# Attention feeding a gated mixer and a channel block: the scores of the second head get PSUM banks of their own

## The reference

```python
    scores = scale * np.matmul(q, k.transpose(0, 1, 3, 2))      # q, k: (4, 8, 576, 64)
    mask = pos[:, None] // 64 >= pos[None, :] // 64
    scores = np.where(mask, scores, -1000000000.0)
    scores = scores - np.max(scores, axis=-1, keepdims=True)
    attn = np.exp(scores)
    attn = attn / (np.sum(attn, axis=-1, keepdims=True) + 1e-09)
    return np.matmul(attn, v)
```

## Time and profile before

| | us |
|---|---|
| median of 3 runs | 778.47 |
| lowest and highest run | 778.45, 778.65 |
| the profiled execution | 780.42 |
| its span, first to last instruction | 778.6 |
| TensorE busy in it | 768.2 |
| mean granted clock of TensorE, share of 2.4 GHz | 0.997 |

### The profile page before, as it was taken

One profiled execution on the slowest core, in us unless ns is written; L12 is line 12 of the kernel. 1 busy time (PEld: TensorE's weight loads), 2 busy tenths in 40 slices (PEclk: granted clock), 3 DMA queues, 4 the chain that ended last, 5 costly groups with the idle time before them and its releaser, 6 DMA issues.

```text
span 778.6 us, 14021 instructions
## 1 busy us (share of the span) xinstructions
PE 768.2 (99%) x5024; PEld 674.3 (87%) x5024; DVE 475.2 (61%) x963; ACT 364.9 (47%) x970; POOL 388.7 (50%) x508
## 2 busy tenths in 40 slices
PE   7999999999999999999999999999999999999998
PEld 6877899779987799879988998888998898889986
DVE  4776745465553755448867676788556687444435
ACT  4886765546554555433543333453423345333431
POOL 3787665234352344313555456465555457454641
PEclk9999999999999999999999999999999999999999
DMA  7344331312214120040362311003100001300002
GB/s 237 135 168 150 106 116 48 102 61 78 77 48 136 41 75 18 21 155 14 122 190 89 114 55 55 28 0 122 55 28 2 1 0 41 122 1 1 0 1 82
DMA packets 38148, 56.38 MB, mean 72 GB/s; under 512 B 3136, under 2 KB 20544, under 8 KB 38080
## 3 DMA queue, kind: packets, MB, share of 16 engines
q1 hardware_dynamic: 38080, 55.49, 22.0%
HBM read 46.04 MB, written 9.44 MB: 71 GB/s over the span
## 4 chain that ended last, share of the span: by engine, by line
PE 97%; DVE 1%; ACT 1%; issue 1%; POOL 0%; POOLq 0%; ACTq 0%; DVEq 0%
PE psum L1393 25%; PE psum L1394 25%; PE psum L1395 25%; PE psum L1306 7%; PE psum L1355 5%; PE psum L1374 3%; PE psum L1379 3%; PE psum L1359 2%; PE psum L1472 1%; ACT probs L808 1%; PE psum L1445 1%; PE psum L1428 1%; DVE neg_max L1035 1%; PE psum L1426 0%; DVE mix_buf L1097 0%
## 5 line engine op out<-in xcount | busy, mean ns | idle before, releaser
L762 POOL TENSOR_TENSOR wp_r<-block,wp_r 128x256 fp32r<-128x256 f32 x168 | 133.8, 804 | 168.3 <-ACT wp_r L939 166.0
L1210 DVE TENSOR_TENSOR sums<-psum,sums 128x384 f32<-128x384 f32 x216 | 113.6, 553 | 105.9 <-PE psum L1395 105.2
L967 ACT ACTIVATE h_r<-sums 128x384 fp32r<-128x384 f32 x96 | 50.4, 525 | 228.9 <-PE psum L1395 119.1
L694 POOL TENSOR_SCALAR probs<-probs,row_inv 128x64 f32<-128x64 f32 (+4 forms) x160 | 87.4, 566 | 111.6 <-DVE row_inv L1046 111.6
L1395 PE MATMUL psum<-w_r,h_r 128*128 128x512 f32 x288 | 114.2, 397 | 0.0
L1394 PE MATMUL psum<-w_r,h_r 128*128 128x512 f32 x288 | 113.7, 395 | 0.0
L1393 PE MATMUL psum<-operand,wp_r 128*128 128x384 f32 x336 | 113.2, 337 | 0.2 <-DVE sums L1210 0.2
L1394 PE MATMUL psum<-operand,wp_r 128*128 128x384 f32 x336 | 113.1, 336 | 0.0
L1395 PE MATMUL psum<-operand,wp_r 128*128 128x384 f32 x336 | 112.4, 334 | 0.0
L1393 PE MATMUL psum<-w_r,h_r 128*128 128x512 f32 x288 | 111.9, 389 | 0.0
L808 ACT ACTIVATE probs<-psum,neg_max 64x64 f32<-64x64 f32 (+4 forms) x160 | 83.0, 527 | 53.7 <-DVE neg_max L1035 52.6
(11 more groups left out here) (121 smaller groups left out, 1592.1 us busy)
## 6 DMA issues: line engine op xcount, KB each, us to landing
qk_raw<-qk SPq DMA_DIRECT2D x32, 576.0 KB, 4.4
block<-w_ch SPq DMA_DIRECT2D x32, 256.0 KB, 4.0
y_res<-y_scratch SPq DMA_DIRECT2D x18, 256.0 KB, 4.1
out<-y_res SPq DMA_DIRECT2D x18, 256.0 KB, 2.1
v_raw<-vN SPq DMA_DIRECT2D x16, 256.0 KB, 2.8
y_scratch<-mix_buf SPq DMA_DIRECT2D x16, 256.0 KB, 2.1
y_ring<-y_scratch SPq DMA_DIRECT2D x16, 256.0 KB, 2.7
w_raw<-w_in SPq DMA_DIRECT2D x8, 256.0 KB, 4.5
```

The source lines that it names most:

```text
L694: pool.tensor_scalar(probs[:, n % 2, c], probs[:, n % 2, c], row_inv[:, n % 2, AT[t]:AT[t] + 1], 1.0, ALU.mult, ALU.mult).then_inc(normed, 1)
L762: pool.tensor_tensor(wp_lo[:, n % WP], w1[i % BLOCKS][:, WEIGHT[j]], wp_hi[:, n % WP].bitcast(F32), ALU.subtract).then_inc(wp_lo_done, 1)
L1210: dve.tensor_tensor(dst, product_bank(i, j), other, ALU.add).then_inc(c_summed, 1)
```

## The change

The scores of head 1 get banks 3 to 5 in place of 0 to 2 (`start += 3 * 512`), and the corner of head 0's own tile moves to bank 6, of head 1's to bank 7. `score_head(1)` is issued right behind `score_head(0)`, and no longer waits for the exponentials of head 0. VectorE sets eight corners in place of four. Behind the two sets of scores come eight identity matmuls with 64 output rows in place of six with 128. The loop issues no scores in head 0's turn.

Two waits are new in the turn of head 0. The transposes of tile 3 go to bank 7, where head 1's own scores lie now, and wait for their exponential. The transposes of tile 2 go to bank 3, and wait for all ten exponentials of heads 0 and 1 (`exped` at 10). Nothing changes from head 2 on, but for the place of the own tile in heads 0 and 1.

```diff
--- before.py
+++ after.py
@@ -344,7 +344,9 @@
 
         def transposed_free(pe, n, t):
 
-            if t == 3 and H < n + 1 < HEADS:
+            if t == 2 and n == 0:
+                pe.wait_ge(exped, 2 * NT)
+            if t == 3 and (n == 0 or H < n + 1 < HEADS):
                 pe.wait_ge(exped, NT * (n + 1) + 1)
             elif t == 2 and n >= H:
                 pe.wait_ge(t_copied_dve, len(DVE_TILES) * n + 1)
@@ -367,13 +369,15 @@
         def score_of(n, t):
             flat = psum.rearrange("p a n -> p (a n)")
             if t == 0:
-                return (m_bank if n <= H else t_bank)[BLOCK:P, 1, 7 * BLOCK:8 * BLOCK]
+                bank = t_bank[:, 0, :] if n == 0 else m_bank[:, 1, :] if 1 < n <= H else t_bank[:, 1, :]
+                return bank[BLOCK:P, 7 * BLOCK:8 * BLOCK]
             start = {4: 0, 3: KEYS[4], 2: KEYS[4] + KEYS[3], 1: KEYS[4] + KEYS[3] + KEYS[2]}[t]
+            start += 3 * 512 if n == 1 else 0
             return flat[:, start:start + KEYS[t]]
 
         def unseen():
 
-            return [score_of(0, t)[0:BLOCK, KEYS[t] - BLOCK:KEYS[t]] for t in TILES[1:]]
+            return [score_of(n, t)[0:BLOCK, KEYS[t] - BLOCK:KEYS[t]] for n in range(2) for t in TILES[1:]]
 
         def parts(t):
             return slice(BLOCK, P) if t == 0 else slice(0, P)
@@ -1315,7 +1319,7 @@
             def score_head(n):
 
                 pe.wait_ge(q_scaled, n + 1)
-                if n >= 1:
+                if n >= 2:
                     pe.wait_ge(exped, NT * n)
                 if n > H:
                     pe.wait_ge(t_copied_act, len(ACT_TILES) * (n - 2) + 2)
@@ -1445,14 +1449,16 @@
                     pe.matmul(t_bank[:, 0, 0:P], ident[:, :], ident[:, :], start=True, stop=True)
 
             keep_warm(10)
-            pe.wait_ge(masks_set, 4)
+            pe.wait_ge(masks_set, 8)
             pe.wait_ge(consts_set, 5)
             score_head(0)
-            keep_warm(6)
+            score_head(1)
+            for _ in range(8):
+                pe.matmul(t_bank[0:BLOCK, 0, 0:P], ident[:, 0:BLOCK], ident[:, :], start=True, stop=True)
             for n in range(HEADS):
                 for step in range(STEPS):
                     if step == 0:
-                        if n + 1 < HEADS:
+                        if 1 <= n < HEADS - 1:
                             score_head(n + 1)
                         if n >= 1:
                             attend(n - 1)
```

## The result

The changed kernel is slower. The median of its 13 runs is 780.55 us (779.65 to 781.63), that of 13 runs of the kernel before beside them 778.65 us (778.35 to 782.17), and the ratio is 1.0019 with a 95% interval of 1.0012 to 1.0027. That is 1.9 us, and outside the range of the prediction (776.5 to 779.9). The runs of before aren't all alike: nine took 778.35 to 779.02 us, and four 780.46 to 782.17, about as long as the runs after the change.

The account below looks back on a forecast made before the run. TensorE, busy 99% of the span, was taken as the bound, with idle stretches and its clock as levers. A chain gain of 0.84 less 0.65 given back left 0.19 us, so 778.47 became 778.3 us; range 776.5 to 779.9.

Parts of the forecast that it names:

- What bounds the kernel, and where the change acts: Whole span: TensorE busy 99%, so only its few idle stretches, two near the start, and its clock can move the time.
- Part 1, the chain: Head 1's scores move up, its wide maximum follows at 12.06, not 12.90; TensorE's release comes 0.84 us earlier.
- Parts 2 and 3, what is given back: Head 0's transposes start at 13.0; seven now stand between the release and head 2's scores, giving back 0.65 us.
- Part 4, filler and masks: Eight identity matmuls behind the first two heads' scores and four more memsets fall in idle time and cost nothing.
- Cost nothing; the cover ends there: Filler ahead of head 0's transposes: even at the slow price it would end at 13.9, transposes at 15.2, before 15.89.
- equal clock: Head 2's scores: the clock falls at about the same place as before, leaving 0.19 us gained, 778.3 us; chance 0.58.
- rival B: Head 2's scores: the change puts there a fall that unprofiled runs of before lack; 1.47 us slower, 779.9 us; chance 0.15.
- Rival A: Head 2's scores: the clock no longer falls and they take 2.03 us; gain 1.85 us, 776.6 us; chance 0.18.

Follow-up runs that it names:

- experiment 4: Kernel before with only the wait for all ten exponentials added ahead of head 0's tile 2 transposes; median 779.35 us, ratio 1.0014.
- experiment 6: Changed kernel plus five identity matmuls in bank 0 between the first three tiles' transposes and the wait for all exponentials; median 778.96 us, ratio 0.9995.
- Experiment 5: Changed kernel with twelve in place of eight identity matmuls behind the scores of heads 0 and 1; median 780.18 us, ratio 1.0010.
- 1: Kernel before with twelve for six identity matmuls behind head 0's scores and four behind head 0's transposes; median 778.84 us, ratio 0.9997.
- 2: Changed kernel with twelve for eight identity matmuls ahead of head 0's transposes and five in bank 0 before the wait; median 778.29 us, ratio 0.9993.
- 7: Changed kernel with both idle stretches filled and eight in place of ten identity matmuls at the start; median 778.22 us, ratio 0.9989.
- 9: Kernel before with both idle stretches filled and eight in place of ten identity matmuls at the start; median 778.52 us, ratio 0.9999.
- 11: Changed kernel, idle stretches filled, eight matmuls at the start, weight loads queued behind head 5's and 6's q and k loads; median 778.07 us, ratio 0.9985.
- the tenth kernel: Kernel before without the six identity matmuls behind head 0's scores; median 778.82 us, ratio 1.0006.

## Why the prediction was wrong, point by point

**What bounds the kernel, and where the change acts.** Right. All of it lies ahead of head 3's scores: the rest takes 755.1 us before and after.

**Part 1, the chain.** Right in mechanism and size. VectorE's program order kept the own maximum of head 1 at 4.15 us behind the wide maxima of head 0 (12.19 less 8.04), before 4.16 (11.83 less 7.67). The release came 9.06 - 8.23 = 0.83 us earlier, forecast 0.84.

**Parts 2 and 3, what is given back.** Right in mechanism, the size a little small. The first transposes wait for the normalised tile until 13.43, 13.06 without the shift of 0.37, forecast 13.0. The seven transposes cost 17.01 - 16.27 = 0.74 us, forecast 0.65, and 0.73 to 0.76 in experiment 4. The prediction took 0.12 us for each of the two wide ones out of a pipelined row of ten; behind a wait the two take 0.34 until the next group can start. The net gain is 0.83 - 0.74 = 0.09 us, forecast 0.19.

**Part 4, filler and masks.** The filler took 1.96 us in idle time, as worked out, and the eight memsets 0.63, forecast 0.66:

```profile
0.80 0.63 DVE L1018 MEMSET psum<- 64x64 f32 x8 [0.80 <-PEq L1550]
```

But the step "Cost nothing; the cover ends there" priced filler by TensorE's time alone. The gap that it leaves open costs more: with five more matmuls there (experiment 6) the median is 778.96 us against 780.55, on another chip, and no fall is left.

**The step that failed: the clock.** The prediction saw that the stretch from 12.2 to 16.54 was thinner than before, and forecast a fall over the scores of head 2. It came, in 13 of 13 runs by their mean clock, and at that place in the one that was traced. The step that failed is the next one: it took the same fall for the runs of before, because the profiled execution had one, and on that set "equal clock" at 0.58. In fact 17 of 110 runs of before have a fall, and the profiled execution, at a mean clock of 0.997, was of that kind. So the case was rival B, at 0.15: the change puts the fall there. The number that decided it stood in the prediction: 780.42 for the profiled execution against 778.47 for the median, 1.95 us. The runs of before with a fall are also 1.95 us above those without. Rival B named this reading and set against it that profiling may simply cost that. The three runs that lay within 0.2 us of each other were, by their length, all without a fall (778.45 to 778.65; no run of before with one is under 780.43), and the argument used them for "one state in all of them", and then chose the wrong state.

**The size of B.** It was priced at 1.66 - 0.19 = 1.47 us, from the one group of scores in the trace. Measured are 1.95 between the two groups of runs, and 1.9 between the medians of before and after: 1.95 less 0.09. The price of the fall itself was not too low. From the start of head 2's scores to that of head 3's it is 6.80 us in the trace of before (23.53 less 16.73) and 6.81 in the changed kernel's, and 5.26 in the sixth's, which has no fall: 1.55 us. Some 0.4 of the 1.95 therefore lies elsewhere. From head 3's scores on these traces agree (755.1 us with a fall, 777.4 - 22.40 = 755.0 in the sixth). What differs from one execution to the next is the start. In the ten traces with ten matmuls at the start the wide maxima of head 0 begin anywhere from 6.99 to 8.32 us. Whether executions with a fall are also those that start late isn't shown, so where the 0.4 us lie stays open. Some runs after have more low time than one fall (mean clocks of 0.995 and 0.996, 6 to 8 us at the lower level), and these are the three longest, 781.00 to 781.63 us. By the fall and the gain alone, 1.55 less 0.09, the median would be 778.65 + 1.46 = 780.1; the rest, up to 780.55, is that unexplained part. The range ended at 779.9, B's own likeliest time, and so left no room above B.

**Rival A** (no fall) names a real mechanism at the wrong place. Its argument was the long busy stretch that ends at 12.2. Experiment 5 makes that stretch longer and still has a fall in 10 of 12 runs; experiment 6 adds five matmuls behind it and has none.

## What to carry to other kernels

Before a change near an idle stretch of TensorE is priced, find out whether the profiled execution has a fall of the clock and whether the runs have one: a profiled time that is off the median by about the price of a fall is a sign that they differ. A wait moved in front of light work can cost little by the chain and still, with what else moves, bring a fall of the clock in every run, so price a schedule by where TensorE's idle time lies and not only by its sum. Work that nobody reads is worth adding where it stands in front of a wait, ends before the release, and most runs have a fall to lose: it gave 1.6 to 2.3 us in the changed kernel and nothing in the median of the kernel before.

## What the runs showed of the hardware

- The same kernel has falls of the clock in some executions and none in others: 17 of 110 before, 13 of 13 after the change, 0 of 70 in the six kernels with the second gap filled or both (1, 2, 6, 7, 9 and 11). By the durations the rise at the start varies as well: the ten matmuls there took 3.98 us in one execution and 4.64 in seven of ten, and the seven score records of head 0 behind them 1.34 to 2.14 us. The Trainium skill (TensorE: Matmul & The Clock Gate, § What's actually happening) says that the place of the change varies from run to run; these runs agree, by 0.66 us in the ten matmuls alone.
- A fall can cost nothing: four runs of the tenth kernel at a mean clock of 0.998, some 3 us at the lower level, took no longer than its runs at 1.00. No trace of these was taken, so that the low stretch lay over idle time there is argued and not shown.
- Two matmuls right behind a wait take 0.34 us until the next group starts, and as part of a row of ten 0.25 us.
- A load of q and k issued at 25.87 us was there for the scaling at 31.16, one issued at 27.90 only for the scaling at 34.71. Both stood behind one weight load on the queue. Why the second took 1.5 us longer wasn't followed.
